# An attention and gated-mixer kernel: weight product and first dense tiles issued between attention's matmuls, block sums of v kept on chip, keys in one padded buffer

## The reference, cut to what matters

```python
# attention, per batch and head; block = 32, window = 16
k_sum = k.reshape(B, H, nb, block, D).max(axis=3)
v_sum = v.reshape(B, H, nb, block, D).mean(axis=3)
scores = concat([where(|i - j| < window, scale * q @ k.T, -1e9), scale * q @ k_sum.T + log(block)])
x = softmax(scores) @ concat([v, v_sum])          # then heads side by side: (B, S, 512)
# layer 1
h = relu(x @ w_in); u, v = halves(h); v_n = layernorm(v)
g = u * (w_spatial @ v_n + b_spatial[:, None])
y = g @ w_out
# layer 2
h2 = relu(y @ w_in2)                              # kernel: g @ (w_out @ w_in2)
c = depthwise convolution of h2 over the sequence, 3 taps
out = (h2 * sigmoid(c)) @ w_out2
```

## Time and profile before

| what | us |
|---|---|
| median of 3 runs | 374.37 |
| lowest, highest | 374.15, 376.27 |
| the profiled execution, whole | 374.59 |
| its span, first to last instruction | 372.6 |
| PE busy in the span | 350.8 (94%) |
| DVE, ACT, POOL busy | 223.2, 138.2, 73.0 |

### The profile page before, as it was taken

The page is one execution under the profiler, slowest core; times in us unless marked ns, Lnnn a source line. Parts: engine busy times, 40 slices in busy tenths (PEclk is TensorE's granted clock), DMA queues, the critical chain, the costliest instruction groups (busy, mean ns, idle before and its releaser), DMA issues.

```text
span 372.6 us, 6760 instructions
## 1 busy us (share of the span) xinstructions
PE 350.8 (94%) x2613; PEld 312.4 (84%) x2613; DVE 223.2 (60%) x572; ACT 138.2 (37%) x398; POOL 73.0 (20%) x87
## 2 busy tenths in 40 slices
PE   6598686989999999999999999999999999999996
PEld 6377565868889889999999988999999988889984
DVE  2759688596258367247644462368775557756662
ACT  3848577484255336341111122421222123122111
POOL 4314456364000000069100094000000000000000
PEclk9969899699999999999999999999999999999999
DMA  9999789864000201365100000000000003100004
GB/s 180 202 186 193 180 193 190 166 157 103 5 0 3 84 1 24 111 201 174 56 2 0 2 0 0 2 0 2 1 0 2 0 0 115 55 2 1 0 2 169
DMA packets 51604, 25.75 MB, mean 69 GB/s; under 512 B 44252, under 2 KB 46580, under 8 KB 51572
## 3 DMA queue, kind: packets, MB, share of 16 engines
q1 hardware_dynamic: 51572, 25.32, 29.1%
HBM read 20.98 MB, written 3.15 MB: 65 GB/s over the span
## 4 chain that ended last, share of the span: by engine, by line
PE 83%; DVE 5%; SPq 4%; issue 3%; ACT 2%; DMA 1%; ACTq 0%; DVEq 0%
PE bank L868 24%; PE bank L870 24%; PE bank L869 24%; PE bank L853 3%; ACT P L487 2%; PE bank L805 2%; PE bank L841 2%; DVE pT L628 2%; DVE SM L648 1%; PE bank L813 1%; SPq L277 1%; PE bank L909 1%; SPq L270 1%; PE bank L831 1%; DMA vw<-vs_s 1%
## 5 line engine op out<-in xcount | busy, mean ns | idle before, releaser
L870 PE MATMUL bank<-g_h,W_l 128*128 128x384 f32 x128 | 43.0, 336 | 0.0
L869 PE MATMUL bank<-g_l,W_h 128*128 128x384 f32 x128 | 42.9, 335 | 0.0
L868 PE MATMUL bank<-g_h,W_h 128*128 128x384 f32 x128 | 42.8, 334 | 0.0
L487 ACT ACTIVATE P<-SM,nmax 128x120 f32<-128x120 f32 x96 | 36.7, 384 | 12.6 <-DVE nmax L648 12.0
L870 PE MATMUL bank<-wo_h,hg_l 128*128 128x512 f32 x96 | 38.0, 396 | 0.0
L869 PE MATMUL bank<-wo_l,hg_h 128*128 128x512 f32 x96 | 38.0, 396 | 0.0
L868 PE MATMUL bank<-wo_h,hg_h 128*128 128x512 f32 x96 | 37.9, 395 | 0.0
L414 POOL TENSOR_TENSOR P<-P,rinv 128x480 f32<-128x480 f32 x24 | 23.7, 987 | 45.9 <-DVE rinv L635 45.9
L868 PE MATMUL bank<-wsT_h,vn_h 128*128 128x384 f32 x96 | 32.2, 335 | 0.0
L869 PE MATMUL bank<-wsT_l,vn_h 128*128 128x384 f32 x96 | 32.1, 334 | 0.0
L870 PE MATMUL bank<-wsT_h,vn_l 128*128 128x384 f32 x96 | 32.1, 334 | 0.0
(11 more groups left out here) (111 smaller groups left out, 803.5 us busy)
## 6 DMA issues: line engine op xcount, KB each, us to landing
stage<-in_moe_w_in SPq DMA_DIRECT2D x8, 512.0 KB, 4.3
vw<-in_v SPq DMA_DIRECT2D x16, 240.0 KB, 4.8
kn<-in_k SPq DMA_DIRECT2D x16, 192.0 KB, 3.6
qn<-in_q SPq DMA_DIRECT2D x16, 192.0 KB, 4.1
stage<-in_moe_w_out SPq DMA_DIRECT2D x6, 512.0 KB, 3.6
out<-obuf SPq DMA_DIRECT2D x12, 256.0 KB, 2.0
stage<-in_moe_w_spatial SPq DMA_DIRECT2D x6, 384.0 KB, 3.9
vw<-vs_s SPq DMA_DIRECT2D x32, 36.0 KB
```

The source lines that it names most:

```text
L487: a.activation(P[:, i % NP_, j, :], SM[:, i % 2, j, :], ACT.Exp, bias=nmax[:, c:c + 1], scale=-1.0, accum_out=rsum[:, c:c + 1]).then_inc(e ...
L868: t_.matmul(dst, lhs[0](c), rhs[0](c), start=first, stop=False)
L869: t_.matmul(dst, lhs[0](c), rhs[1](c), start=False, stop=False)
L870: ins = t_.matmul(dst, lhs[1](c), rhs[0](c), start=False, stop=last)
```

## The change

In the parts that the prediction speaks of:

1. Fills. PE's slots 1 to 27 get dense tiles between the scores and the values product (`fills_at`): the transposes of w_out in slots 1 and 2; the 8 W tiles in slots 5, 6, 7, 8, 9, 11, 13 and 15; batch 0's 6 v tiles in slots 17 to 22 and its 8 u tiles in slots 23, 24, 25 (two), 26 (two) and 27 (two). ACT and DVE empty them in the same slots. After attention batch 1's v, u and w_spatial's transposes come, then the s tiles, then at once layer 2.
2. PSUM: units and fills share a ring of 4 banks; scores keep 2; transposed probabilities and values products have one bank each in place of two.
3. Block sums of v: a small selecting product (`("vp", p, 0)`, one matmul a pair) puts the 24 sums on partitions 96 to 119, DVE copies them, and POOL spreads them over the 12 tiles of `vw` (`spread_sums`). The 32 DMAs are gone.
4. Keys: `kT` holds the transposed keys once, with 16 zero columns at each end. Scores are two matmuls in place of one for each tile and head: 96 columns from `kT` and 24 from `ks`. DVE's three copies a pair are gone.
5. Weights: 3 stage buffers in place of 4; order w_out, w_in2, w_in, w_spatial, w_out2. SP loads three of them before v of pair 1. POOL splits w_in2 and w_in in 24 parts between the multiplications of slots 1 to 15.
6. ACT's queue loads q of the first two pairs. DVE writes the masked scores into `P` itself. POOL in place of ACT and DVE splits v_n. Intermediate tiles of g and v are kept whole in place of three rotating buffers.

```diff
-    NVB, NP_, NST = 3, 4, 4
+    NVB, NP_, NST = 3, 4, 3
+    SLOTS = NG + 5
-        TR, SC, PTB, OT = bank[0:2], bank[2:4], bank[4:6], bank[6:8]
+        SC, PTB, OT = bank[4:6], bank[6], bank[7]
+        units_at[-1] = [("k", 0, 0), ("k", 0, 1), ("q", 0, 0), ("q", 0, 1)]
+            units_at[GP * p] += [("k", p + 1, 0), ("k", p + 1, 1)] if more else []
+            units_at[GP * p] += [("vs", p, 0)]
+            units_at[GP * p + 1] += [("q", p + 1, 0), ("q", p + 1, 1)] if more else []
+            units_at[GP * p + 1] += [("vp", p, 0)]
+        fills_at[1] = [("wo", 0), ("wo", 1)]
+        fills_at[2] = [("wo", 2), ("wo", 3)]
+        for n, i in enumerate((5, 6, 7, 8, 9, 11, 13, 15)):
+            fills_at[i] = [("W", n % FC, n // FC)]
+        b0 = [("v", 0, m) for m in range(SC6)] + [("u", 0, f, n) for f in range(FC) for n in range(2)]
+        for n, i in enumerate((17, 18, 19, 20, 21, 22, 23, 24, 25, 25, 26, 26, 27, 27)):
+            fills_at[i].append(b0[n])
+        items = [("wo", 0), ("wo", 1)] + [("w2", n, c) for n in range(2) for c in range(KC // 2)]
+        items += [("wi", c) for c in range(KC)] + [("ws", c) for c in range(SC6)] + [("wo2", c) for c in range(GC // 2)]
```

SP's queue (each load_k and load_q waits until the pair before last's unit has been transposed; load_v(p) waits for `pv_done` of 3(p - 2), that is, until the values product of pair p - 3 is through; a stage load waits for the tile three before it to be used up):

```diff
             load_k(0)
-            load_q(0)
             load_k(1)
-            load_q(1)
             sp.wait_ge(vpads, 2 * NVB)
             load_v(0)
+            for n in range(NST):
+                load_item(n)
             load_v(1)
-            sp.wait_ge(tr_done, tr_count(("k", 0, 1)))
             load_k(2)
-            sp.wait_ge(tr_done, tr_count(("q", 0, 1)))
             load_q(2)
+            load_v(2)
+            n = NST
             for p in range(NP):
                 if p + 3 < NP:
                     load_k(p + 3)
+                if n < 9:
                     load_item(n)
                     n += 1
+                if p + 3 < NP:
+                    load_q(p + 3)
+                if 0 < p and p + 2 < NP:
+                    load_v(p + 2)
+                if p < 2 or 4 <= p:
+                    load_item(n)
+                    n += 1
```

POOL in attention (`split_part(n)`: of each weight tile of 128 x 1024 part 0 waits for its DMA and makes the high half of all 1024 columns, parts 1 and 2 make the low parts of 512 each):

```diff
+            parts = iter(range(3 * 2 * KC))
+            for i in range(1, SLOTS):
                 n = i - 1
+                if n < NG:
+                    pool.wait_ge(rinv_ready, n + 1)
+                    pi = P[:, n % NP_, :, :]
+                    g.tensor_tensor(out=pi, in0=pi, in1=rinv[...], op=ALU.mult).then_inc(norm_done, 1)
+                if i % GP == 2 and i // GP < NP:
...
+                    spread_sums(i // GP)
+                for _ in range(1 if i % GP == 2 else 2):
+                    part = next(parts, None)
+                    if part is not None:
+                        split_part(part)
```

PE:

```diff
                 for h in range(2):
-                    at = h * KA
-                    for odd in range(2):
+                    for lo, n in ((0, KW), (KW, NB)):
+                        for odd in range(2):
...
+                                keys = kT[rows, p % 2, t * TQ:t * TQ + KW] if lo == 0 else ks[rows, p % 2, :]
+                                ins = t_.matmul(SC[e][odd * TQ:(odd + 1) * TQ, h * KA + lo:h * KA + lo + n],
+                                                qT[rows, p % 2, t * TQ:(t + 1) * TQ], keys, start=True, stop=True)
+            for i in range(SLOTS):
                 if 3 <= i < NG + 3:
                     transpose_probs(i - 3)
                 if i < NG:
                     scores(i)
-                else:
-                    mix(next(early))
-                if i >= 4:
+                for u in units_at[i]:
+                    unit(u)
+                for u in fills_at[i]:
+                    dense(u)
+                if 4 <= i < NG + 4:
                     values(i - 4)
-            for u in early:
-                mix(u)
+            for u in seq[ATT:]:
+                dense(u)
```

More of the change, by code:

```diff
@@ new lines, in attention_mixer_program, with bank_no @@
+        seq += [("v", 1, m) for m in range(SC6)]
+        seq += [wst.pop(0) for _ in range(4)]
+        for f in range(FC):
+            for n in range(2):
+                seq += [("u", 1, f, n), wst.pop(0)]
+        seq += [("cw",)]
+        S_AT = len(seq)
+        for b in range(B):
+            seq += [("s", b, f, n) for f in range(FC) for n in range(2)]
+        place = {u: n for n, u in enumerate(seq)}
+        def bank_no(n):
+            return n % 4 if n < ATT else (4 + n - ATT) % 8
@@ new lines, in split_part @@
+            def split_part(n):
+                j, part = divmod(n, 3)
+                if j < KC:
+                    h, c = divmod(j, KC // 2)
+                    x, done = ("w2", h, c), w2_split
+                    cols = slice(h * 512, (h + 1) * 512)
+                    high = w2_h[:, 2 * c:2 * c + 2, cols]
+                    row = 2 * c + (part - 1)
+                    halves = (w2_h[:, row, cols], w2_l[:, row, cols]) if part else None
+                else:
+                    c = j - KC
+                    x, done = ("wi", c), wi_split
+                    high = wi_h[:, c, :].rearrange("p (j m) -> p j m", j=2)
+                    cols = slice((part - 1) * 512, part * 512)
+                    halves = (wi_h[:, c, cols], wi_l[:, c, cols]) if part else None
+                if part == 0:
+                    split_high(x, high)
+                else:
+                    split_low(x, part - 1, *halves, done)
@@ new lines, in _ @@
+            for t in range(B * SC6):
+                b, m = divmod(t, SC6)
+                pool.wait_ge(vn_ready, t + 1)
+                g.tensor_copy(vn_h[b][:, m, :], vraw[b][:, m, :]).then_inc(vnh_ready, 1)
+                pool.wait_ge(vnh_ready, t + 1)
+                g.tensor_tensor(out=vn_l[b][:, m, :], in0=vraw[b][:, m, :], in1=vn_h[b][:, m, :].bitcast(fp32),
+                                op=ALU.subtract).then_inc(vnl_ready, 1)
+            pool.wait_ge(gated, 2 * FC)
+            for c in range(GC // 2):
+                x = ("wo2", c)
+                stage_wait(pool, x)
+                rows = slice(2 * c, 2 * c + 2)
+                src = stage[:, item[x] % NST, :]
+                high = wo2_h[:, rows, :].rearrange("p j m -> p (j m)")
+                n_hi += 1
+                g.tensor_copy(high, src).then_inc(split_hi, 1)
+                pool.wait_ge(split_hi, n_hi)
+                g.tensor_tensor(out=wo2_l[:, rows, :].rearrange("p j m -> p (j m)"), in0=src, in1=high.bitcast(fp32),
+                                op=ALU.subtract).then_inc(wo2_split, 1)
@@ new lines, in _ @@
+            for u in units_at[-1]:
+                take_unit(u)
+            for i in range(SLOTS):
+                if i >= 5:
+                    n = i - 5
+                    p, r = divmod(n, GP)
+                    b, c0 = p // PPB, r * GT * TQ
+                    dve.wait_ge(xh_ready, n + 1)
+                    vv.tensor_tensor(out=x_l[b][:, p % PPB, c0:c0 + GT * TQ], in0=OT[:, 0:GT * TQ],
+                                     in1=x_h[b][:, p % PPB, c0:c0 + GT * TQ].bitcast(fp32),
+                                     op=ALU.subtract).then_inc(xl_ready, 1)
@@ new lines, in _ @@
+            for m in range(SC6 + 1):
+                t = SC6 + m
+                if m < SC6:
+                    v_stats(t)
+                if m >= 1:
+                    dve.wait_ge(std_ready, 1 + m)
+                    vv.reciprocal(rstd[:, t - 1:t], std[:, t - 1:t]).then_inc(rstd_ready, 1)
+                    dve.wait_ge(rstd_ready, 1 + m)
+                    v_norm(t - 1)
+            for u in seq[ATT:S_AT]:
+                if u[0] == "ws":
+                    take_fill(u)
+            src = out_of_ring(("cw",))
```

745 lines of the change are left out of this document (323 added, 422 removed).

## The result

The changed kernel takes 391.96 us (median of 4 runs), the kernel before beside it 374.50: ratio 1.0458, 95% interval 1.0422 to 1.0493. The forecast was 388.0, in a range from 376 to 397. The profiled execution took 392.21, its span is 390.5.

What follows compares the result with a forecast made beforehand. Attention was taken as paced by loads, with PE time left in it. 374.6 plus 12.3 (batch 1 starting at 160.1 against 147.8) plus 1.1 (s tiles waiting for w_spatial's split) gave 388.0 us, range 376 to 397.

Steps and rivals of the forecast that it cites:

- Slot 5: Before W's first matmul: PE idles 7.6 us for w_in2's split, lower clock costs 2.0 more; W starts at 36.1.
- Slot 16: Before group 13's transposes: PE idles 9.3 us behind w_in's last tile and POOL, lower clock costs 2.0.
- Scores in two pieces: Attention's scores: 16 more instructions a group cost 0.28 us, making 0.85; bounds nothing and 0.57.
- some 5 us of extra score instructions: Attention's PE-bound slots: 18 groups at 0.28 extra, 5.0 us in all.
- Small groups and dense tiles in turn: Slots 5 to 27: fills priced as back to back, 2.74 us a v or W tile, 2.08 a u tile.
- Batch 1's start and the s tiles: After attention: 1.2 us wait for the last group's split, then 1.1 for w_spatial's split before the s tiles.
- Layer 2's edge: Layer 2's start behind the s tiles, waiting for ACT and DVE to finish g: 0, in a range to 2.
- The weights are there in time: Rival for slots 5 and 16: both waits and both clock losses go, 367.1 us; chance 0.12.
- the first wait: Slot 5's wait for W's weights, 7.6 us idle and 2.0 of lower clock.
- the second: Slot 16's wait for w_in's last tile, 9.3 us idle and 2.0 of lower clock.
- Only the first wait goes: Rival for slot 5: DMA faster or W's parts early, so that wait vanishes, 378.4 us; chance 0.15.

Runs made afterwards that it cites:

- e2: Changed kernel with w_in's last tile loaded ahead of v of pair 6 and the fourth weight tile ahead of v of pair 2: 377.34 us, 1.0093.
- e4: Changed kernel with batch 0's six v tiles taken out of slots 17 to 22 and put behind attention: 396.36 us, 1.0607.
- e1: Changed kernel with w_in's last tile loaded right behind k of pair 7, ahead of v of pair 6: 382.44 us, 1.0225.
- e7: e6 with the block keys' 24 columns multiplied for two query tiles at once, 4 products a group for 8: 379.81 us, 1.0137.
- e3: Changed kernel with scores in one product of 120 columns again, block keys left out: 390.29 us, 1.0433.
- e10: e6 with batch 0's first eight dense tiles two to a slot (18, 20, 22, 24): 376.72 us, 1.0070.
- e6: e2 with two s tiles ahead of batch 1's v tiles, a u tile behind the last s tile, bank ring shifted by one: 374.34 us, 0.9988.
- e9: e8 with pair 0's second sums product two steps earlier, ahead of pair 1's key transposes: 366.11 us, 0.9774.
- e8: Kernel before with v's block sums on chip and keys in one padded buffer, no dense tile moved: 371.81 us, 0.9922.
- e5: Kernel before with only v's block sums kept on chip, no DMAs for them: 374.39 us, 0.9997.

## Why the prediction was right

Right was the direction, and the mechanism at both places; the sum was 4 us short. That it is no further off is partly luck: scores priced 2.9 too dear stand against some 7.5 us of other work priced too low. Step by step:

- **Slot 5.** Forecast: W starts at 36.1, slot 6 at 41.4. Measured: 35.70, and its transposes at 41.59. The fourth tile landed at 31.06 (31.0 forecast). These times come out because the weights' way sets them. PE's own side did not: slot 5's scores were done at 31.7 and not at 28.5, after small waits and slow products in slots 0 to 4 that I had not priced (six transposes of q at 15.88 are 1.34 long), so the wait was 4.00 and not 7.6. The lower clock cost 5.27 for the tile instead of 2.96, 2.3 us (2.0). Both are 6.3, not 9.6, and e2 takes off 5.1: it reaches W only at 33.58, behind another stretch at the lower clock (the values at 30.46 are 1.12 long). Its wait of 3.01 for vw at 13.41, as against 0.73 in the kernel after, is not the early tile's doing: e4 has the old order and waits 2.83, and v's sums start at 13.2 to 13.4 in all of these kernels.
- **Slot 16.** Forecast: 9.3 idle from 90.8, and 2.0 for the clock. Measured: 8.51 from 92.9, and transposes of 1.10 instead of 0.65 behind it (granted clock 0.72 in 100 to 110 us). From slot 16's transposes to batch 1 it takes 61.05 us, 59.32 in e2, so the clock cost 1.7. e1 gives back 9.5 of these 10.2.
- **Scores in two pieces: over-sized.** I took 0.28 a group, measured are 0.69 - 0.57 = 0.12 (e7's first fence, or 42.17 to 42.86 in the kernel after), and e3 puts all of them at 1 to 2 us, where 0.28 would have made some 5. So PE does not carry "some 5 us of extra score instructions", as I had summed up, but about 2. My bounds were zero and 0.57; the pace of starts that I took from the earlier trace rows does not hold for short products: eight of them follow each other in 0.09, 11 ns each. The Trainium skill's floor of about 25 ns between starts (TensorE: Matmul & The Clock Gate, "Wait — 56ns, not 53.3ns?") is not what this trace shows for 64 x 64 tiles, four of which share the array; for e7's 64 x 128 tiles, 0.56 / 8 = 70 ns, the trace agrees with it.
- **Small groups and dense tiles in turn: the terms that failed.** I priced a tile as back to back ones, 2.74 and 2.08. This is one of them in slot 6 of the kernel after (PE):

```profile
44.46 0.50 PE L874 MATMUL bank<-w_h,woT_h 128*128 128x512 f32 x1
44.79 0.40 PE L875 MATMUL bank<-w_l,woT_h 128*128 128x512 f32 x1
45.03 0.40 PE L876 MATMUL bank<-w_h,woT_l 128*128 128x512 f32 x1
...
47.11 0.39 PE L876 MATMUL bank<-w_h,woT_l 128*128 128x512 f32 x1
47.42 0.39 PE L866 MATMUL bank<-pT,vw 120*64 120x64 f32 x6
```

  The first step is 0.33 where the others are 0.23, and behind the last one the values start after 0.31: 2.96 in all, 0.2 more than 2.74. The same prices stand between small groups of unlike shape: k's transposes take 0.80 (42.86 to 43.66) where v's sums follow, forecast 0.71. The Trainium skill says that TensorE drains when it changes its tiling mode (TensorEngine Tiling (Array Packing), Key Properties); that agrees, and e10 measures 0.19 a place. For the 18 slots 6 to 27 with dense tiles that makes 3.8 us, and k's and q's transposes add 1.1. Transposes of probabilities behind a values product take 0.58; my 0.53 was read behind k's transposes (71.34 to 71.93 in the kernel before shows 0.59): 0.8 more in all. And `vp`, which I put at 0.07 each, takes 0.33, six times 0.26 or 1.6 more:

```profile
67.37 0.40 PE L822 MATMUL bank<-vs_s,psel 128*24 128x128 f32 x2
67.70 0.69 PE L866 MATMUL bank<-pT,vw 120*64 120x64 f32 x16
```

  These are 7.3, less 0.16 x 18 = 2.9 that the scores were too dear: 4.4. Waits and clock came 1.7 under their price (the largest is 8.51 for 9.3 in slot 16), slot 6 started 0.2 late, and the values took 0.2 more. That is 3.1 of the 3.3 by which batch 1's first tile is late: 163.38 where 160.1 was forecast.
- **Batch 1's start and the s tiles.** The wait for x_l is 0.94 (1.2 forecast), the one ahead of s 0.97 (1.1).
- **Layer 2's edge.** I took 0, in a range to 2; it is 0.74 idle. Between 388.0 and the profiled execution's 392.21 lie 4.2 us; 3.3 are named above, and this edge is most of the other 0.9. The wait ends with VectorE's read of the last s tile (L740), which lay in a bank that layer 2 needs at once. e6 takes this and the other two edges away: 3.0 us.
- **The rivals.** "The weights are there in time" was to give 367.1; it is e2, and it gives 377.3. Of the 10.2 between, 4.0 are what the sum itself was short, 4.5 the first wait, priced at 9.6 and worth 5.1, and 1.8 the second, priced at 11.3 and worth 9.5. "Only the first wait goes" was worked out as 378.4; no run has it, but with 5.1 for that wait it would be about 387, an estimate. Taking away the second alone gave 382.4.

Where the expected gain went. Filling the gaps of the earlier trace rows was to bring TensorE's idle time in attention back. The gaps had two other owners: the sums' way over DMA, which the change itself removes, and the first pair's start. With sums and keys on chip and the first spread early, PE is busy 9.40 of 10 us between 50 and 60 us without a dense tile there (e9's span is 363.9, PE busy 349.9). What remains to fill is 0.58 us a pair, and one dense tile costs 0.2 for its place. e6, which has the tiles too, is 8.2 us slower than e9: its PE is busy 356.8. Of these 6.9 us the places are about 4 by the price above, and a stretch at lower clock early on (0.66 in 10 to 20 us, 1.00 in e9) is the likely rest. This split is argued: no run here has e9 with dense tiles alone, and e6 differs from e9 also in its single banks, its order of weights and GpSimd's splits.

## What to carry to other kernels

Before independent work is put into an engine's gaps, find each gap's owner and see whether it can be removed, because filled and removed are not worth the same: here two small parts of the change, with one product moved earlier, gave 2.3%, and the whole change with its edges covered gave nothing. Whether the dense tiles alone take it away was not run. When a step is moved earlier, follow its load through the queue that issues it and its preparation through the engine that does it in order; one load behind one wait held TensorE for 8.5 us. When such a part goes to another engine, count what it adds there (0.3 us a pair on VectorE, and more beside GpSimd's copy). And a price read from back-to-back work doesn't hold between small groups of another shape.

## What the runs showed of the hardware

- A change of shape on TensorE cost about 0.1 us each way at full clock (0.33 for the first step of a dense tile where others take 0.23; 0.19 a place by e10).
- 24-column products with 64 x 64 stationary tiles, four of which lie side by side, start 11 ns apart (eight in 0.09 us); with 64 x 128 tiles and half as many instructions they start 70 ns apart (e7). In a group that is 0.56 us for 0.28: fewer, larger instructions were twice as dear here.
- Idleness is paid again in clock. In e8 PE waits 1.85 us for k at 17.6, and the granted clock is 0.50 from 18 to 28 us; in e9 the same wait is 1.01 and the clock stays at 1.00. With the 2.54 us wait behind it gone too, the next values come 4.97 earlier, 1.6 of it by the clock.
- Removing one bound of 10.7 us a pair (43.30 to 54.04 in the kernel before) showed the next at 9.37 and then 8.95 (e5, e8), with VectorE busy for 8.98 and 8.17 of it. A pair in the kernel before whose sums came in time took 8.45, with VectorE busy for 8.14. So some of the load that VectorE has in e5 came with the new way of the sums; how much of the period that is, no run shows.
